# Bucketed attention with two MLP stages: the division by the denominators moved from ScalarE to GpSimd, and one small copy from VectorE to ScalarE

## What is computed

```python
q_bits = (np.einsum('bhsd,dk->bhsk', q, proj) > 0)
k_bits = (np.einsum('bhsd,dk->bhsk', k, proj) > 0)
mask = q_bucket[:, :, :, None] == k_bucket[:, :, None, :]
scores = scale * np.matmul(q, k.transpose(0, 1, 3, 2))
scores = np.where(mask, scores, -1000000000.0)
attn = np.exp(scores - np.max(scores, axis=-1, keepdims=True))
attn = attn / (np.sum(attn, axis=-1, keepdims=True) + 1e-09)
out = np.matmul(attn, v)
# then, per batch of 768 tokens x 512:
# relu(x @ w_in) split in u, v; v normalised, times w_spatial over tokens, + b; (u * v) @ w_out
# then y + relu(norm(y) * g @ w_ch1) @ w_ch2
```

## Time and profile before

| what | value |
|---|---|
| median of 3 runs | 697.5 us (696.96 to 697.53) |
| the profiled execution, its own time | 695.97 us |
| its span on the engines | 694.1 us |
| granted TensorE clock, mean | 0.998 |
| PE, PEld busy | 675.4 us (97%), 600.3 us (86%) |
| DVE busy | 360.0 us (52%) |
| ACT busy | 296.8 us (43%) |
| POOL busy | 303.9 us (44%) |

### The profile page before, as it was taken

The page is one execution under the profiler, slowest core; times in us unless marked ns, Lnnn a source line. Parts: engine busy times, 40 slices in busy tenths (PEclk is TensorE's granted clock), DMA queues, the critical chain, the costliest instruction groups (busy, mean ns, idle before and its releaser), DMA issues.

```text
span 694.1 us, 11979 instructions
## 1 busy us (share of the span) xinstructions
PE 675.4 (97%) x3815; PEld 600.3 (86%) x3815; DVE 360.0 (52%) x828; ACT 296.8 (43%) x681; POOL 303.9 (44%) x312
## 2 busy tenths in 40 slices
PE   6799999999999999999999999999999999999998
PEld 3688888888888898999899999997899899999996
DVE  4899999999999974534621111115524641111113
ACT  3688888888888883411311111112321331111110
POOL 5888777887555516100044444433000024544441
PEclk9999999999999999999999999999999999999999
DMA  6543444543222002100012111104000002111112
GB/s 243 184 123 114 117 133 135 136 167 123 91 91 92 24 4 82 31 0 1 1 56 65 60 60 60 60 30 151 31 1 1 0 32 61 60 60 60 60 60 92
DMA packets 18955, 51.30 MB, mean 74 GB/s; under 512 B 2736, under 2 KB 4912, under 8 KB 18928
## 3 DMA queue, kind: packets, MB, share of 16 engines
q1 hardware_dynamic: 17584, 45.45, 20.6%
q0 software_dynamic: 1344, 5.51, 2.4%
HBM read 47.75 MB, written 3.19 MB: 73 GB/s over the span
## 4 chain that ended last, share of the span: by engine, by line
PE 70%; issue 13%; DVE 12%; DVEq 1%; ACT 1%
PE bank L716 13%; PE bank L742 12%; PE bank L490 8%; PE bank L492 8%; PE bank L491 7%; PE bank L721 6%; PE bank L746 6%; DVE PTl L991 6%; DVE negated L971 3%; PE bank L540 3%; DVE Q L944 1%; PE bank L509 1%; PE bank L508 1%; PE bank L554 1%; PE bank L552 1%
## 5 line engine op out<-in xcount | busy, mean ns | idle before, releaser
L1105 DVE SCALAR_TENSOR_TENSOR Hl<-bank,Hh 128x384 fp32r<-128x384 f32 x64 | 35.7, 558 | 208.9 <-ACT Hh L872 208.5
L366 POOL TENSOR_SCALAR W1h<-w_raw 128x512 fp32r<-128x512 f32 x32 | 19.9, 622 | 279.0 <-PE bank L721 224.4
L872 ACT ACTIVATE Hh<-bank 128x384 fp32r<-128x384 f32 x64 | 31.5, 492 | 216.1 <-PE bank L721 216.1
L811 ACT ACTIVATE Pe<-bank,neg_max 128x768 f32<-128x768 f32 x96 | 86.9, 905 | 31.2 <-DVE negated L971 30.8
L971 DVE TENSOR_SCALAR_CACHE_REDUCE negated<-bank 128x768 bf16<-128x768 f32 x96 | 91.6, 954 | 15.2 <-PE bank L509 11.7
L991 DVE TENSOR_TENSOR PTl<-bank,PTh 128x384 fp32r<-128x384 f32 x192 | 97.7, 549 | 2.3 <-ACT PTh L806 1.8
L540 PE MATMUL bank<-cst,Pe 128*128 128x128 f32 x576 | 86.1, 282 | 9.3 <-DVE PTl L991 9.2
L806 ACT ACTIVATE PTh<-bank 128x384 fp32r<-128x384 f32 x192 | 86.2, 493 | 8.5 <-PE bank L540 8.2
L540 PEld LDWEIGHTS bank<-cst,Pe 128*128 128x128 f32 x576 | 65.1, 141 | 26.6 <-DVE PTl L991 13.5
L716 PE MATMUL bank<-XNh,W1l 128*128 128x384 f32 x256 | 86.9, 340 | 0.0
L716 PE MATMUL bank<-XNh,W1h 128*128 128x384 f32 x256 | 86.7, 339 | 0.0
(11 more groups left out here) (130 smaller groups left out, 1338.5 us busy)
## 6 DMA issues: line engine op xcount, KB each, us to landing
w_raw<-w_ch SPq DMA_DIRECT2D x32, 512.0 KB, 3.5
q_raw<-qqT SPq DMA_DIRECT2D x16, 384.0 KB, 5.0
k_raw<-kkT SPq DMA_DIRECT2D x16, 384.0 KB, 5.5
qk_raw<-qkT SPq DMA_DIRECT2D x15, 384.0 KB, 3.1
v_raw<-v SPq DMA_DIRECT2D x16, 192.0 KB, 4.4
out<-X SPq DMA_DIRECT2D x12, 256.0 KB, 2.1
rows<-code_rows SPq DMA_DIRECT2D x15, 192.0 KB, 4.4
w_raw<-w_spT POOLq DMA_DIRECT2D x6, 384.0 KB, 3.3
```

Of the source, the lines that this page charges most:

```text
L811: nc.scalar.activation(Pe[n % 2][:, :].rearrange("p (c n) -> p c n", c=2), bank[:, 2 * (n % 2):2 * (n % 2) + 2, 0:C], ACT.Exp, bias=neg_ma ...
```

## The change

- `scale_o` (ScalarE): three activations with `scale=rden[...]` become one plain copy of 128 x 384 from PSUM to `On`. It no longer waits for the reciprocals.
- `sum_halves` (GpSimd): the sum of the halves is written back into `On`, and a second instruction multiplies it by `rden`, broadcast over the 64 columns, into `X`. It waits for the sum (`x_summed`) and for the reciprocals (`rden_done`). `x_done` is now counted up by the multiply.
- `inverse` (VectorE): waits in addition until the multiply that used this half of `rden` before is done.
- `copy_codes`: from VectorE to ScalarE, each time behind the rounding of the same step (n = 2, in the first head n = 1; the first one behind the first exponentials). Its wait for the earlier store (`row_out`) moves with it. ScalarE's loop over pairs of heads is cut as VectorE's was, so that the last pairs have no codes.

```diff
@@ sum_halves
-                nc.gpsimd.tensor_tensor(X[:, b, HC * m:HC * (m + 1), h * D:(h + 1) * D],
-                                        On[:, :, 0:D], On[:, :, D:2 * D], ALU.add).then_inc(x_done, 1)
+                nc.gpsimd.tensor_tensor(On[:, :, 0:D], On[:, :, 0:D], On[:, :, D:2 * D], ALU.add).then_inc(x_summed, 1)
+                pool.wait_ge(x_summed, 2 * hh + m + 1)
+                pool.wait_ge(rden_done, 2 * hh + m + 1)
+                nc.gpsimd.tensor_tensor(X[:, b, HC * m:HC * (m + 1), h * D:(h + 1) * D], On[:, :, 0:D],
+                                        rden[:, m, :].unsqueeze(2).to_broadcast([P, HC, D]),
+                                        ALU.mult).then_inc(x_done, 1)
@@ scale_o
                 act.wait_ge(x_done, START + cc)
-                act.wait_ge(rden_done, cc + 1)
+                passed(act)
                 act.wait_ge(o_turned, cc + 1)
-                for t in range(HC):
-                    last = nc.scalar.activation(On[:, t, :], bank[:, MISC, t * P:(t + 1) * P], ACT.Copy,
-                                                scale=rden[:, c % 2, t:t + 1])
-                last.then_inc(o_scaled, 1)
+                nc.scalar.activation(On[:, :, :], bank[:, MISC, 0:C].rearrange("p (t d) -> p t d", t=HC),
+                                     ACT.Copy).then_inc(o_scaled, 1)
+            def copy_codes(n, s):
+
+                act.wait_ge(codes_mm, n)
+                nc.scalar.activation(codes[s][0:2 * G, :], bank[0:2 * G, MISC, CODES_AT:CODES_AT + W],
+                                     ACT.Copy).then_inc(buckets, 1)
@@ ScalarE's steps, at the end of step n
+                    if first and n == 1:
+                        copy_codes(2, 0)
+                    elif hashed and n % T == 2:
+                        act.wait_ge(row_out, ROW_START + 16 * (hh0 + n // T))
+                        passed(act)
+                        copy_codes(hh0 + n // T + 2, (n // T) % 2)
@@ ScalarE's stream
             exps(0, 0)
-            steps(0, range(4), first=True)
-            with act.Fori(0, NP - 1) as pair:
-                steps(pair, range(4, TILES + 4))
-            steps(NP - 1, range(4, TILES), last=True)
+            copy_codes(1, 1)
+            steps(0, range(4), False, first=True)
+            with act.Fori(0, NP - 2) as pair:
+                steps(pair, range(4, TILES + 4), True)
+            steps(NP - 2, range(4, TILES), True)
+            steps(NP - 2, range(TILES, TILES + 4), False)
+            steps(NP - 1, range(4, TILES), False, last=True)
@@ VectorE: copy_codes and its three calls are gone; inverse
             def inverse(cc0, c):
+                dve.wait_ge(x_done, START + cc0 + c - 1)
+                passed(dve)
                 dve.wait_ge(den_done, START + cc0 + c + 1)
```

More of the change, by code:

```diff
@@ L217, in bucket_attention_mlp_kernel @@
         rden_done = sem("rden_done")
+        x_summed = sem("x_summed")
         x_done = sem("x_done")
@@ L821, in scale_o, with steps @@
                 act.wait_ge(x_done, START + cc)
-                act.wait_ge(rden_done, cc + 1)
+                passed(act)
                 act.wait_ge(o_turned, cc + 1)
-                for t in range(HC):
-                    last = nc.scalar.activation(On[:, t, :], bank[:, MISC, t * P:(t + 1) * P], ACT.Copy,
-                                                scale=rden[:, c % 2, t:t + 1])
-                last.then_inc(o_scaled, 1)
-            def steps(pair, which, last=False, first=False):
+                nc.scalar.activation(On[:, :, :], bank[:, MISC, 0:C].rearrange("p (t d) -> p t d", t=HC),
[4 more added lines that the diff above has]
+                                     ACT.Copy).then_inc(buckets, 1)
+            def steps(pair, which, hashed, last=False, first=False):
                 g0, cc0, hh0 = TILES * pair, 4 * pair, 2 * pair
@@ L978, in make_bits @@
                 nc.vector.tensor_scalar(bits[s][:, :], bank[:, MISC, 0:W], 0.0, 1.0, ALU.is_gt, ALU.mult).then_inc(bits_made, 1)
[L980 to L984, removed]
             def pt_lo(g, n):
@@ L1019, in steps @@
                         make_bits(2, 0)
-                    elif first and n == 1:
-                        copy_codes(2, 0)
                     elif hashed and n % T == 1:
                         make_bits(hh0 + n // T + 2, (n // T) % 2)
[L1024 to L1027, removed]
                     if coding and n == (1 if first else n // T * T):
@@ L1186, in _ @@
             maximum(1, 1)
-            copy_codes(1, 1)
             steps(0, range(4), False, first=True)
```

## The result

The changed kernel took 700.09 us (median of 4 runs, 699.2 to 700.99) beside 697.23 for the kernel before (4 runs, 696.67 to 697.53): a ratio of 1.0047, 95% interval 1.0034 to 1.006, so slower by 2.9 us where 5.7 were forecast. The profiled execution took 699.2 us with a span of 697.4 (before: 695.97 and 694.1).

The account below looks back on a forecast made before the run. The prediction took a VectorE-TensorE loop in the attention heads as the bound. GpSimd's later splits holding off the key one-hot cost 6.0 us, less 0.3 at attention's end: +5.7, median 697.5 to 703.2 us, range 697.5 to 707.

Parts of the forecast that it names:

- The coupling: VectorE's key one-hot waits for an overlapping GpSimd instruction to finish, then takes 0.41 us.
- The multiply, x: GpSimd's added 128x192 multiply in each half: 0.67 us more, bounds 0.56 and 1.0.
- ScalarE's shorter copy: One copy of 0.48 us replaces three scalings of 0.88; GpSimd's later sum in a head starts 0.40 us sooner.
- The shift of the split: GpSimd's residual split of a weight piece starts 2 x 0.67 - 0.40 = 0.94 us later relative to VectorE.
- W_sp heads: Six attention heads in which GpSimd splits a w_spatial piece; key one-hot forecast +0.63 us each, 3.8 us.
- W_in heads: Early heads in which GpSimd splits a w_in piece; two already blocked ones forecast +0.94 us each, 1.9 us.
- The first W_in head: Head with the w_in piece at 36.62 us, before which no multiply has run: forecast +0.27 us.
- The terms set to zero: Codes' copy leaving VectorE and joining ScalarE, and the reciprocal's wait on VectorE: each taken as 0 us.
- The start and the end: Attention's start: first codes' copy, 0 (-0.1 to +0.4 us); its end: VectorE's shorter wait for ScalarE, -0.3 us.
- fast rival: GpSimd late enough for VectorE's key one-hot to go first: faster, 695.9 us, chance 0.06.
- third rival: One-hot shares with GpSimd's split or the multiply is cheap: within 0.2%, 696.9 to 698.5 us, chance 0.13.
- The second: Rival: VectorE's copy of the codes was on the path: -3.5 us, 694.0 us, chance 0.03.

## Why the prediction came out as it did

The mechanism held at each step, and the price of it was too high: +5.7 forecast, +2.9 in the medians, 3.3 in the profiled executions. The time fell into the range, in its lower half; the forecast of the cost itself was twice what came.

- **The coupling.** Right. The one-hot ends 0.42 after the 128x768 split of GpSimd (0.41 forecast from the W_in rows), and the three kernels with extra sums show the rule in both directions.
- **The multiply, x.** Too high. A sum and the wait behind it are 0.66 from start to start (113.94 to 114.60), as the forecast had it. But the multiply takes 0.51 and occupies 0.47, where the forecast put a sum's row, 0.59 and 0.56. The broadcast operand, feared as a cost, came out cheaper. Sum and multiply together hold GpSimd for 1.13 (113.94 to 115.07) where the sum alone held it for 0.56: x = 0.57 instead of 0.67, at the lower bound. For that bound (0.56) the prediction's sum of the heads was 4.1, and 4.0 was measured.
- **ScalarE's shorter copy.** 0.43 sooner instead of 0.40: the sum of step 3 starts 2.10 after that step's transposes (119.95 to 122.05) where it was 2.53 (117.48 to 120.01), and the kernel without the multiply shows the same 0.43.
- **The shift of the split.** This is the term that was mis-sized. Twice the multiply's 0.10 and ScalarE's 0.03 come together in it: 0.94 forecast, 2 x 0.57 - 0.43 = 0.71 by the terms as measured, 0.74 by the split's end itself (from 0.10 ahead of the one-hot's start to 0.64 behind it). Of it the W_sp heads pay 0.74 less the 0.30 that the margin and the 0.62 allow, 0.44 in the one-hot and 0.40 in the head. Forecast 0.63 a head and 3.8 us, measured 2.4. The W_in heads were already blocked and pay the whole shift: 0.72 and 0.75 against 0.94. The first W_in head paid 0.07 against 0.27. Together 4.0 measured for 6.0.
- **The terms set to zero.** Right, all of them: the codes' copy off VectorE (wait 0.48 to 0.72, 0.73 forecast; put back, no difference), the copy on ScalarE (0.30, inside its wait), the reciprocal's new wait (heads without a piece 15.08 as before, and nothing lost without the multiply).
- **The start and the end.** The end gave -0.35 for -0.3, of which the wait for ScalarE makes 0.26. The start gave -0.31 in the profiled pair, with the clock of the one execution in it. It can't be set against the change.
- **The rivals.** The fast rival, in which GpSimd is late enough to let the one-hot go first, was a real one: four extra sums bring it about, at +0.7. But it was priced too well: it let the early heads lose most of their 0.4 us as well, and there the one-hot met the rounding ahead of the split and took 1.3. The change is far from it: its W_sp split starts 1.19 ahead of the one-hot (115.99 to 117.18), so each multiply would have to cost 0.60 more. The third rival, that the shift is absorbed, is refuted by one-hots of 1.06. The second, that the codes' copy was on the path, is refuted here; with the one-hot moved, the heads of 14.79 against 14.54 speak for it.

What the forecast did not look for is how cheaply the loss could be undone. It took the place of the one-hot as given. VectorE's wait of 0.48 at step 4 was named as cover for the codes, and it is also a place to put the one-hot in: that one line is worth some 12 us (ratio 0.9874 against the changed kernel's 1.0047).

## What to carry to other kernels

Moving work to an idle engine is priced by what it shifts on that engine, not by its busy share: look which of its instructions will then lie across a fast instruction of VectorE on the loop, since one extra sum cost 3.0 us, two 9.4 and four 0.7. Where two such instructions meet, let the one that nobody waits for come second, or move the one on the loop into a wait that the engine has anyway. An edit that frees time inside a wait is worth nothing until something is moved there: the same change that lost 2.9 us gained 2.3 once the one-hot stood in that place (and V was split last in both kernels).

## What the runs showed of the hardware beyond what was expected

- The issue of a DMA by GpSimd (0.58 us) also holds VectorE's one-hot off, but not for its whole length: 0.23 us of overlap cost 0.17 in one kernel (114.17 to 114.40), 0.34 cost 0.08 in another (114.31 to 114.65), and in the kernel with the one-hot a step later 0.43 cost 0.32 (71.13 to 71.56). Which part of the issue does it stays open.
- GpSimd loses as VectorE does when it comes second, all but 0.13 to 0.15 us of the overlap (VectorE: all but 0.2): the sum 0.59 to 0.98, the multiply 0.51 to 0.85, the 128x768 split 1.84 to 2.06, the split of V 1.00 to 1.28.
- A multiply of GpSimd with one operand broadcast along its last dimension took 0.51 for 128x192, less than the sum of two full operands (0.58 to 0.60).
- The one-hot with an accumulator took 1.01 us for 64x768, the queries' one of the same size 1.28, with another reading pattern and other operations.
